# Fused block-sparse attention, top-2 expert attention and token/channel mixer on one core: the guard of the softmax sums, the first key loads, and the scaling of half the queries are rearranged

## The chip, the cores and the metric

The kernel runs on one core of one Trainium2 chip. The metric is the device time of one execution in microseconds. Before the change it is 440.44 us (median of 3 runs, 440.24 to 440.9). All data is float32, and the tolerance is tight enough that the large products are computed as three passes over a high and a low part of each operand.

## The reference

Three stages run one after the other on two batch entries (B = 2, 768 tokens, 8 heads of 64).

```python
# 1: each token attends to its neighbours and to one summary per block of 32 keys
k_sum = k.reshape(B, H, nb, block, D).max(axis=3)          # nb = 24, block = 32
v_sum = v.reshape(B, H, nb, block, D).mean(axis=3)
scores_l = scale * q @ k.T          # kept where |i - j| < 16, else -1e9
scores_s = scale * q @ k_sum.T + log(block)
a = exp(concat(scores_l, scores_s) - rowmax)
a = a / (sum(a) + 1e-9)
x = a @ concat(v, v_sum)
# 2: four experts of causal attention over x, top 2 of 4 by a gate, each projected and summed
# 3: a mixer over tokens (768 -> 256 -> 768), added, then over channels (512 -> 1536 -> 512), added
```

`scale` is 1/8, a power of two, so it is exact wherever it is applied: on the keys or on the queries.

## The kernel before

The program is written engine by engine; the order of the text is the order on each engine, and semaphores are the only coupling. There are five instruction streams: PE (matmul), DVE (vector), ACT (scalar), POOL (GpSimd) and SP, which issues nearly all DMAs.

**Attention, first stage.** For each batch entry `b` there are 12 steps `u`. Steps 0 to 5 take the six tiles of 128 queries for the first two pairs of heads (pairs 0 and 1, `q = 0`), steps 6 to 11 the same tiles for pairs 2 and 3 (`q = 1`). One step goes through:

- `a_scores` on PE: mask, then `QT` (queries, transposed) against `KW`. `KW[:, pair, window, :]` holds for every window of 64 queries its 96 neighbouring keys and the 24 block maxima, already multiplied by `scale`.
- `a_maxima` on DVE (L1464): the negated row maximum `nmaxA`.
- `a_exps` on ACT (L1192): four exponentials, each with its row sum in `sumA`.
- `a_maxima` again on DVE, one step later: `denA` = `sumA` + 1e-9 (L1469), then its reciprocal (L1475).
- `normalise` on POOL (L601): `PA` times the reciprocal, 128x480.
- `a_transpose` on PE, then `a_to_sbuf` to `PTA` (on ACT for even steps, on DVE for odd, L1482), `a_values` on PE, `a_x_hi` on ACT and `a_x_lo` on DVE (L1488) for the high and low part of the result.

The function `sequence` of each engine interleaves these with a counter `k`: at `k` PE does the scores of step `k`, the transpose of step `k - 3` and the values of step `k - 4`.

**Who builds `KW`.** In the first batch entry the windows of pairs 0 and 1 are copied and scaled on ACT (`first_windows`, L1201) and their block maxima come from DVE (`half_of_key_maxima`, L1606, on halves of the tokens); pairs 2 and 3 are scaled on POOL (`key_window`, L633), three pieces each, placed between the `normalise` calls by the table `KEY_COPIES`, and their maxima are written by DVE (`key_maxima` L1615, `fill_maxima` L1624). In the second entry pairs 0 and 1 are done on POOL during the expert stage of the first entry. `COPY_BEHIND` says after which `normalise` POOL copies block means into `VW` (L651), and `PACED` after which it splits the first weight matrix (`split_step`, L613 and L620).

**The start.** SP loads both halves of pair 0's keys, ACT's queue both halves of pair 1's; then come the first tile of queries, more queries, the keys of pair 2 and the values for the block means (`VT`), all from SP. PE warms up with 12 matmuls on `ident_b`, which POOL has built by then.

The expert stage, the token mixer and the channel mixer are not touched, except that POOL has two more instructions in the expert stage of the first entry.

Of the kernel before, what the change touches and what calls it, by code (L numbers as in the profile page):

```python
# [15 lines left out]
P = 128  # L16
# [13 lines left out]
KC = WK + NB  # L30
# [53 lines left out]
N_WARM = 12  # L84
# [9 lines left out]

MEANS_AT = 8

PACED = (5, 5, 7, 7, 8, 8)
# [38 lines left out]
def program(nc, qT_d, kT_d, vw_d, vT_d, wq_d, wk_d, wv_d, wo_d, tok1_d, tok2_d, ch1_d, ch2_d, out_d):  # L136
    with ExitStack() as ctx:
# [23 lines left out]
        sumA = sb("sumA", [P, 4, 4], F32)  # L161
# [13 lines left out]
        gate_s = sb("gate_s", [P, 2, TQ], F32)  # L175
        US1 = [None] * TQ
# [115 lines left out]
        c_mask = sem("c_mask"); c_rows = sem("c_rows")  # L292
# [17 lines left out]
        a_zero = sem("a_zero")  # L310
        a_kfirst = sem("a_kfirst"); a_kfill0 = sem("a_kfill0"); a_kfill = sem("a_kfill")
# [50 lines left out]
        def windows_by(b, q, i):  # L362

            return (2 * b + q - 1) * 6 + (4 + i if b == 0 else 2 * i + 2)

# [43 lines left out]
        def _(sp):  # L409
# [45 lines left out]
            for half in range(2):  # L455
                load_half_of_keys(sp, 0, half)
# [96 lines left out]
        def _(pool):  # L553
# [70 lines left out]
            def key_window(b, r, i):  # L624

                if i == 0:
# [6 lines left out]
                pool.tensor_scalar(KW[:, r, 4 * i:4 * i + 4, 0:WK], windows(r, 4 * i), SCALE, None,  # L633
                                   ALU.mult).then_inc(a_kwin, 1)
# [75 lines left out]
            for b in range(B):  # L710
# [25 lines left out]
                for t in range(TQ):  # L736
# [20 lines left out]
        def _(pe):  # L757
# [4 lines left out]
            pe.wait_ge(c_pool, 2)  # L762
            for _ in range(N_WARM):
                mm(bank[0], ident_b[:, :], ident_b[:, :].unsqueeze(1).broadcast_to([P, 4, P]), True, True)
# [4 lines left out]
            def a_scores(b, u):  # L769
# [10 lines left out]
                if t % 2 == 0:  # L780
# [16 lines left out]
                for j in range(2):  # L797
                    pair = 2 * q + j
                    if b + u == 0:
                        pe.wait_ge(*((a_kfirst, 1) if j == 0 else (a_kfill0, 1)))  # L800
# [323 lines left out]
            for k in range(3):  # L1124
                a_scores(0, k)
                for _ in range(WARM_BEHIND[k]):
                    mm(ps_o[:, :], ident_b[:, :], ident_b[:, :].unsqueeze(1).broadcast_to([P, 4, P]), True, True)
# [58 lines left out]
        def _(act):  # L1186
            def a_exps(b, u):
# [3 lines left out]
                for j in range(4):  # L1191
                    last = act.activation(PA[:, u % NPA, j, :], ps_s[u % 2][:, j % 2, (j // 2) * KC:(j // 2 + 1) * KC],  # L1192
                                          ACT.Exp, bias=nmaxA[:, u % 4, j:j + 1],
                                          accum_out=sumA[:, u % 4, j:j + 1])
                last.then_inc(a_exp, 1)

            def first_windows(i):
                for r in range(2):
# [207 lines left out]
            for half in range(2):  # L1406
# [463 lines left out]
```

## Time and profile before

| | |
|---|---|
| median of 3 runs | 440.44 us |
| the profiled execution's own time | 440.58 us |
| its span | 438.7 us |
| PE busy | 427.5 us, 97% |
| DVE busy | 291.0 us, 66% |
| ACT busy | 227.6 us, 52% |
| POOL busy | 144.1 us, 33% |

The shares are averages over stages with different limits. In the page's forty slices, slice 1 (the first 11 us) and the slices up to about 33 us are those where PE is least busy while DVE and ACT are at 7 to 9 tenths; after them PE is at 9 tenths almost throughout. The granted TensorE clock is at full speed in all forty slices. The profiled execution took 1.9 us more than its span; that part lies outside what the trace shows.

### The profile page before, as it was taken

Reading aid. Unit: us, or ns where it says so; the run is one execution under the profiler, and the core shown is the slowest. Engines: PE = TensorE matmul, PEld = TensorE weight load, DVE = VectorE, ACT = ScalarE, POOL = GpSimd, SP = SyncE. Lnnn points to the kernel's source line nnn. Section 1 sums busy time; section 2 is a strip of 40 time slices with the busy share of each in tenths; the row PEclk is TensorE's granted clock in tenths of the full one; section 3 lists DMA queues with packets and bytes.
Section 4 is the critical chain, followed back from the end, with each engine's and each line's share of the span. In section 5 each row is a group of like instructions: output and inputs, shape, how many; then the busy total and the mean of one; then the engine's idle time right before and its main releaser. Section 6 shows DMA issues by size and latency. Waiting matters only on the chain.

```text
span 438.7 us, 8549 instructions
## 1 busy us (share of the span) xinstructions
PE 427.5 (97%) x3327; PEld 364.5 (83%) x3327; DVE 291.0 (66%) x518; ACT 227.6 (52%) x581; POOL 144.1 (33%) x162
## 2 busy tenths in 40 slices
PE   7889999999999999999999999999999999999996
PEld 3669996887767799878877998998898999889885
DVE  4983569786478535776867875876765765575353
ACT  6895567774259736876856353434443233323120
POOL 5898927000038510001195464333122022200000
PEclk9999999999999999999999999999999999999999
DMA  8954370000870500000033013113113152301103
GB/s 282 367 203 139 108 289 0 1 2 1 291 293 13 164 6 2 0 1 1 11 105 127 1 49 96 49 48 97 48 49 96 70 184 83 97 0 49 48 0 145
DMA packets 14799, 39.66 MB, mean 90 GB/s; under 512 B 1656, under 2 KB 3368, under 8 KB 14760
## 3 DMA queue, kind: packets, MB, share of 16 engines
q1 hardware_dynamic: 14328, 38.60, 26.3%
q8 instruction: 27, 0.44, 0.4%
q10 hardware_dynamic: 432, 0.52, 0.4%
q14 instruction: 12, 0.10, 0.1%
HBM read 33.56 MB, written 4.72 MB: 87 GB/s over the span
## 4 chain that ended last, share of the span: by engine, by line
PE 87%; DVE 6%; ACT 4%; issue 2%; DMA 1%; SPq 0%; DVEq 0%
PE ps_s L759 35%; PE ps_o L759 19%; PE ps_x L759 15%; PE ps_t L759 11%; PE ps_t L941 4%; ACT PA L1192 3%; DVE nmaxA L1464 1%; DMA KP<-in_kT 1%; DVE PTA L1482 1%; DVE vsum L1630 1%; PE ps_x L958 1%; PE ps_t L835 1%; DVE denA L1469 1%; DVE XT_l L1488 0%; PE ps_s L1032 0%
## 5 line engine op out<-in xcount | busy, mean ns | idle before, releaser
L1443 ACT ACTIVATE HID_h<-HID_raw 128x384 fp32r<-128x384 f32 x48 | 25.1, 525 | 72.4 <-DVE HID_raw L1799 32.1
L704 POOL TENSOR_TENSOR W_raw<-W_raw 128x256 f32<-128x256 f32 x11 | 11.7, 1067 | 98.2 <-DMA W_raw<-in_ch 88.2
L601 POOL TENSOR_TENSOR PA<-PA,denA 128x480 f32<-128x480 f32 x24 | 23.8, 990 | 49.4 <-DVE denA L1475 49.3
L1192 ACT ACTIVATE PA<-ps_s,nmaxA 128x120 f32<-128x120 f32 x96 | 33.7, 382 | 9.9 <-DVE nmaxA L1464 9.8
L759 PE MATMUL ps_s<-C_h,HID_l 128*128 128x512 f32 x96 | 37.8, 393 | 0.0
L759 PE MATMUL ps_s<-C_l,HID_h 128*128 128x512 f32 x96 | 37.7, 393 | 0.0
L759 PE MATMUL ps_s<-C_h,HID_h 128*128 128x512 f32 x96 | 37.7, 392 | 0.0
L1558 DVE TENSOR_REDUCE nmaxM<-ps_s 128x1 f32<-128x640 f32 (+5 forms) x28 | 26.7, 955 | 12.8 <-PE ps_s L759 12.7
L1788 DVE SCALAR_TENSOR_TENSOR HID_l<-HID_raw,HID_h 128x384 fp32r<-128x384 f32 x48 | 28.0, 587 | 10.7 <-ACT HID_h L1443 8.4
L1264 ACT ACTIVATE PM<-ps_s,nmaxM 128x128 f32<-128x128 f32 (+5 forms) x48 | 30.1, 633 | 5.6 <-DVE nmaxM L1558 5.3
L759 PE MATMUL ps_o<-V_h,W_h 128*128 128x384 f32 x96 | 32.8, 342 | 0.1
L759 PE MATMUL ps_o<-V_h,W_l 128*128 128x384 f32 x96 | 32.4, 338 | 0.0
L759 PE MATMUL ps_o<-V_l,W_h 128*128 128x384 f32 x96 | 32.3, 337 | 0.0
L1664 DVE TENSOR_TENSOR W_l<-W_raw,W_h 128x1792 fp32r<-128x1792 f32 x12 | 26.1, 2179 | 5.4 <-ACT W_h L1329 5.4
L1437 ACT ACTIVATE U<-ps_o 128x384 f32<-128x384 f32 x12 | 5.9, 492 | 40.0 <-PE ps_o L759 40.0
L759 PE MATMUL ps_x<-V_h,W_h 128*128 128x384 f32 x72 | 24.3, 338 | 0.0
L759 PE MATMUL ps_x<-V_l,W_h 128*128 128x384 f32 x72 | 24.2, 336 | 0.0
L759 PE MATMUL ps_x<-V_h,W_l 128*128 128x384 f32 x72 | 24.2, 336 | 0.0
L941 PE MATMUL ps_t<-ident,PM 128*128 128x128 f32 x168 | 23.3, 275 | 0.9 <-issue 0.4
L1569 DVE COPY PTM<-ps_t 128x512 f32<-128x512 f32 x28 | 19.1, 683 | 7.0 <-PE ps_t L941 6.8
L759 PE MATMUL ps_s<-KH,QS 128*128 128x512 f32 (+3 forms) x64 | 23.6, 374 | 0.0
L1795 DVE TENSOR_TENSOR U<-ps_x,U 128x384 f32<-128x384 f32 x12 | 6.7, 556 | 24.6 <-PE ps_x L759 24.6
(257 smaller groups left out, 1266.0 us busy)
## 6 DMA issues: line engine op xcount, KB each, us to landing
VW<-in_vw SPq DMA_DIRECT2D x12, 512.0 KB, 7.7
W_raw<-in_ch SPq DMA_DIRECT2D x12, 512.0 KB, 3.5
C_raw<-in_ch SPq DMA_DIRECT2D x12, 512.0 KB, 3.9
VT<-in_vT SPq DMA_DIRECT2D x8, 384.0 KB, 7.6
out_x<-US SPq DMA_DIRECT2D x11, 256.0 KB, 2.0
QT<-in_qT SPq DMA_DIRECT2D x7, 384.0 KB, 6.8
KP<-in_kT SPq DMA_DIRECT2D x6, 384.0 KB, 7.0
raw<-in_tok SPq DMA_DIRECT2D x4, 384.0 KB, 3.1
```

The lines of the kernel that those rows point to most:

```text
L601: pool.tensor_tensor(PA[:, u % NPA, :, :], PA[:, u % NPA, :, :], denA[:, u % 2, 1, :].unsqueeze(2).broadcast_to([P, 4, KC]), ALU.mult).the ...
L704: pool.tensor_tensor(W[S3], W[A11], W[A21], ALU.subtract).then_inc(w_sum, 1)
L759: return pe.matmul(out, lhsT, rhs, start=start, stop=stop)
L941: last = pe.transpose(ps_t[:, at_ // 512, at_ % 512:at_ % 512 + P], PM[:, u % 3, at_:at_ + P], ident[:, :])
L1192: last = act.activation(PA[:, u % NPA, j, :], ps_s[u % 2][:, j % 2, (j // 2) * KC:(j // 2 + 1) * KC], ACT.Exp, bias=nmaxA[:, u % 4, j:j + ...
L1264: last = act.activation(PM[:, u % 3, part], ps_s[u % 2][:, :, :].rearrange("p a c -> p (a c)")[:, part], ACT.Exp, bias=nmaxM[:, t, e:e + 1 ...
L1443: act.activation(*own(s, n, half), ACT.Relu).then_inc(g_hi, 1)
L1558: dve.tensor_reduce(nmaxM[:, t, experts[0]:experts[0] + n], ps_s[u % 2][:, :, :].rearrange("p a c -> p (a c)")[:, 0:n * stride] .rearrange ...
L1569: dve.tensor_copy(PTM[u % 3][:, 0:width], ps_t[:, 0, 0:width]).then_inc(m_pt0, 1)
L1664: dve.tensor_tensor(W_l[i][:, :, :, :], W_raw[i][:, :, :, :], W_h[i][:, :, :, :].bitcast(F32), ALU.subtract).then_inc(w_lo, 1)
L1788: dve.scalar_tensor_tensor(HID_l[s % 2][:, n, part], quarter(s, i), 0.0, HID_h[s % 2][:, n, part].bitcast(F32), ALU.max, ALU.subtract).the ...
L1795: dve.tensor_tensor(U2[:, :], Y, U1[:, :], ALU.add).then_inc(g_u2, 1)
```

## The change

Seven edits, in the order of the program:

- **Guard.** `sumA` gets a second column that is set to 1e-9 once; `sumA + 1e-9` is now a sum over two columns (`tensor_reduce`) and no longer a `tensor_scalar`.
- **Keys of the first pairs by halves on both queues.** SP loads the first halves of pairs 0 and 1, ACT's queue the second halves. ACT scales the first window piece of pair 0, writes pair 0's block maxima, and only then scales pair 1's first piece. PE waits for each pair's piece apart.
- **Queries of pairs 2 and 3 scaled, their keys copied.** `KW` of pairs 2 and 3 is a plain copy (on POOL and, for the block maxima, on DVE). The factor goes into `QT[:, 1]`, in two halves of 128x768: on DVE in the first entry (at `k` = 5 and 8), on POOL in the second (in the expert stage of the first).
- **POOL's order.** `KEY_COPIES`, `COPY_BEHIND` and `PACED` move.
- **Warm-up.** A tile `warm`, set by DVE's first instruction, takes the place of `ident_b`, and there are 11 matmuls and no longer 12.

```diff
-KEY_COPIES = (((2, 0, -1), (2, 1, -1), (2, 2, 0), (3, 0, 2), (3, 1, 4), (3, 2, 6)),
+KEY_COPIES = (((2, 0, -1), (2, 1, -1), (2, 2, -1), (3, 0, 3), (3, 1, 4), (3, 2, 4)),
-COPY_BEHIND = (1, 3)
+COPY_BEHIND = (2, 3)
-N_WARM = 12
+N_WARM = 11
+SCALED_AT = (5, 8)
-PACED = (5, 5, 7, 7, 8, 8)
+PACED = (5, 5, 6, 7, 8, 8)
...
-        sumA = sb("sumA", [P, 4, 4], F32)
+        sumA = sb("sumA", [P, 4, 4, 2], F32)
...
-            for half in range(2):
-                load_half_of_keys(sp, 0, half)
+            for r in range(2):
+                load_half_of_keys(sp, r, 0)
...
+                if r < 2:
+                    pool.tensor_scalar(KW[:, r, 4 * i:4 * i + 4, 0:WK], windows(r, 4 * i), SCALE, None,
+                                       ALU.mult).then_inc(a_kwin, 1)
+                else:
+                    pool.tensor_copy(KW[:, r, 4 * i:4 * i + 4, 0:WK], windows(r, 4 * i)).then_inc(a_kwin, 1)
+
+            def scale_queries(b, half):
+                pool.wait_ge((ld_qf, ld_q)[half][1], b * 16 + 16)
+                part = QT[:, 1, half * GT:(half + 1) * GT, :, :].rearrange("p t j s -> p (t j s)")
+                pool.tensor_scalar(part, part, SCALE, None, ALU.mult).then_inc(a_qs, 1)
...
+                    if b < B - 1 and t in (3, 5):
+                        scale_queries(b + 1, t // 2 - 1)
...
-            pe.wait_ge(c_pool, 2)
+            pe.wait_ge(c_warm, 1)
...
                 if t == 0:
-                    pe.wait_ge(*((ld_qt, 16) if b + q == 0 else (ld_qf[q], b * 16 + 16)))
+                    pe.wait_ge(*((ld_qt, 16) if b + q == 0 else queries_by(b, q, 0)))
...
                 if t == GT:
-                    pe.wait_ge(ld_q[q], b * 16 + 16)
+                    pe.wait_ge(*queries_by(b, q, 1))
...
-            for half in range(2):
-                load_half_of_keys(act, 1, half)
+            for r in range(2):
+                load_half_of_keys(act, r, 1)
...
-            first_windows(0)
+            first_windows(0, (0,))
 
             act.wait_ge(a_ksum, 1)
             act.activation(KW[:, 0, :, WK:KC], ksum[:, 0, :].unsqueeze(1).broadcast_to([P, NW, NB]), ACT.Copy,
                            scale=SCALE).then_inc(a_kfirst, 1)
+            first_windows(0, (1,))
...
-                    dve.tensor_scalar(denA[:, before % 2, 0, :], sumA[:, before % 4, :], 1e-9, None,
-                                      ALU.add).then_inc(a_den, 1)
+                    dve.tensor_reduce(denA[:, before % 2, 0, :], sumA[:, before % 4, :, :], AX.X, ALU.add).then_inc(a_den, 1)
...
+            def scale_queries(half):
+                dve.wait_ge((ld_qf, ld_q)[half][1], 16)
+                part = QT[:, 1, half * GT:(half + 1) * GT, :, :].rearrange("p t j s -> p (t j s)")
+                dve.tensor_scalar(part, part, SCALE, None, ALU.mult).then_inc(a_qs0, 1)
...
+                    if b == 0 and k in SCALED_AT:
+                        scale_queries(SCALED_AT.index(k))
...
+            dve.memset(warm[:, :], 1.0).then_inc(c_warm, 1)
             dve.memset(denA[:, 0, 0, 0:1], 0.0)
+            dve.memset(sumA[:, :, :, 1], 1e-9)
```

`queries_by` gives the semaphore that says the queries are ready: the load's own for pairs 0 and 1, that of the scaling (`a_qs0` in the first entry, `a_qs` in the second) for pairs 2 and 3.

Two places show how the instructions move. The first is DVE in the first batch entry, from the low part of step 0's result (`XT_l`, at `k` = 5) on; `vsum` are the sums of the values of pair 2, `nmaxA` is then the maximum of step 6, the first step that reads the scaled queries. Before:

```order
L1488 TENSOR_TENSOR XT_l<-ps_o,XT_h 128x2x128
L1630 TENSOR_REDUCE vsum<-VT 128x24
L1464 TENSOR_REDUCE nmaxA<-ps_s 128x2x2
L1469 TENSOR_SCALAR denA<-sumA 128x4
L1475 RECIPROCAL denA<-denA 128x4
L1482 COPY PTA<-ps_t 120x512
```

and now:

```order
L1511 TENSOR_TENSOR XT_l<-ps_o,XT_h 128x2x128
L1656 TENSOR_SCALAR QT<-QT 128x768
L1661 TENSOR_REDUCE vsum<-VT 128x24
L1488 TENSOR_REDUCE nmaxA<-ps_s 128x2x2
L1493 TENSOR_REDUCE denA<-sumA 128x4
L1498 RECIPROCAL denA<-denA 128x4
L1505 COPY PTA<-ps_t 120x512
```

The scaling of the first half of the queries stands between the low part and the value sums, and the guard is a reduction.

The second is POOL in the first batch entry, from the first pieces of pair 2's keys on (`PA` is `normalise`, `VW` the copy of the means, `wv_h` and `wv_l` the split of the first weights). Before:

```order
L633 TENSOR_SCALAR KW<-KP 128x4x96 x2
L601 TENSOR_TENSOR PA<-PA,denA 128x480
L633 TENSOR_SCALAR KW<-KP 128x4x96
L601 TENSOR_TENSOR PA<-PA,denA 128x480
L651 COPY VW<-VS 24x512
L601 TENSOR_TENSOR PA<-PA,denA 128x480
L633 TENSOR_SCALAR KW<-KP 128x4x96
L601 TENSOR_TENSOR PA<-PA,denA 128x480
L651 COPY VW<-VS 24x512
```

and now:

```order
L649 COPY KW<-KP 128x4x96 x3
L613 TENSOR_TENSOR PA<-PA,denA 128x480 x3
L671 COPY VW<-VS 24x512
L613 TENSOR_TENSOR PA<-PA,denA 128x480
L649 COPY KW<-KP 128x4x96
L671 COPY VW<-VS 24x512
L613 TENSOR_TENSOR PA<-PA,denA 128x480
L649 COPY KW<-KP 128x4x96 x2
```

All three pieces of pair 2 stand ahead of the first `normalise`, so the first three `normalise` calls follow one another; the first piece of pair 3 stands behind the fourth, and its other two behind the fifth.

## Rows read from the trace of the kernel before

**Rows 1.** The page, the chain that ended last, by engine.

```profile
PE 87%; DVE 6%; ACT 4%; issue 2%; DMA 1%; SPq 0%; DVEq 0%
```

**Rows 2.** The chain in order of time, first 52 us: start us, us, what.

```profile
24.12 1.48 ACT PA L1192 x8
...
33.51 1.56 PE ps_s L759 x12
```

**Rows 3.** Timeline of DVE, first entry: start us, us, instruction, [idle before <-releaser].

```profile
5.43 1.47 DVE L1606 TENSOR_REDUCE ksum<-KP 128x12 f32<-128x384 f32 x3 [0.35 <-DMA KP<-in_kT]
6.93 0.31 DVE L1624 TENSOR_SCALAR KW<-ksum 128x288 f32<-128x288 f32 x1
...
9.59 0.95 DVE L1630 TENSOR_REDUCE vsum<-VT 128x24 f32<-128x768 f32 x1 [0.56 <-DMA VT<-in_vT]
...
10.87 0.66 DVE L1464 TENSOR_REDUCE nmaxA<-ps_s 128x4 f32<-128x480 f32 x1
```

**Rows 4.** The same timeline further on, to the last step.

```profile
13.22 0.95 DVE L1469 TENSOR_SCALAR denA<-sumA 128x4 f32<-128x4 f32 x1
...
15.25 0.80 DVE L1624 TENSOR_SCALAR KW<-ksum 128x288 f32<-128x288 f32 x1
...
16.54 0.15 DVE L1469 TENSOR_SCALAR denA<-sumA 128x4 f32<-128x4 f32 x1
...
18.79 0.64 DVE L1464 TENSOR_REDUCE nmaxA<-ps_s 128x4 f32<-128x480 f32 x1
...
19.54 0.18 DVE L1475 RECIPROCAL denA<-denA 128x4 f32<-128x4 f32 x1
19.63 0.40 DVE L1488 TENSOR_TENSOR XT_l<-ps_o,XT_h 128x256 fp32r<-128x256 f32 x1
...
20.80 0.65 DVE L1464 TENSOR_REDUCE nmaxA<-ps_s 128x4 f32<-128x480 f32 x1
...
26.66 0.41 DVE L1488 TENSOR_TENSOR XT_l<-ps_x,XT_h 128x256 fp32r<-128x256 f32 x1
```

**Rows 5.** Timeline of POOL, first entry.

```profile
13.15 0.99 POOL L601 TENSOR_TENSOR PA<-PA,denA 128x480 f32<-128x480 f32 x1
...
15.85 1.23 POOL L633 TENSOR_SCALAR KW<-KP 128x384 f32<-128x384 f32 x1
...
22.89 1.18 POOL L613 CAST wv_h<-raw 128x520 fp32r<-128x520 f32 x2
```

**Rows 6.** Timeline of ACT, first entry: the exponentials of steps 4 and 6.

```profile
16.65 0.36 ACT L1192 ACTIVATE PA<-ps_s,nmaxA 128x120 f32<-128x120 f32 x1 [0.56 <-DVE nmaxA L1464]
...
21.49 0.36 ACT L1192 ACTIVATE PA<-ps_s,nmaxA 128x120 f32<-128x120 f32 x1 [0.27 <-DVE nmaxA L1464]
```

**Rows 7.** Timeline of PE: the warm-up, step 9's mask, the values of step 7.

```profile
1.52 4.85 PE L759 MATMUL ps_s<-ident_b 128*128 128x512 bf16 x12 [1.52 <-POOL ident_b L563]
...
26.83 0.30 PE L759 MATMUL ps_s<-mask_m,ident_b 64*64 64x240 bf16 x4
...
32.23 0.70 PE L759 MATMUL ps_x<-PTA,VW 120*64 120x64 f32 x16 [0.17 <-DVE XT_l L1488]
```

**Rows 8.** Timeline of DVE, second entry.

```profile
133.82 0.94 DVE L1624 TENSOR_SCALAR KW<-ksum 128x288 f32<-128x288 f32 x1
```

**Rows 9.** Timeline of POOL, second entry.

```profile
132.48 1.16 POOL L633 TENSOR_SCALAR KW<-KP 128x384 f32<-128x384 f32 x1
133.61 0.98 POOL L601 TENSOR_TENSOR PA<-PA,denA 128x480 f32<-128x480 f32 x1
```

**Rows 10.** Timeline of ACT, second entry: the exponentials of step 5.

```profile
135.36 0.36 ACT L1192 ACTIVATE PA<-ps_s,nmaxA 128x120 f32<-128x120 f32 x1 [0.32 <-DVE nmaxA L1464]
```

**Rows 11.** Timeline of POOL, expert stage of the first entry.

```profile
67.47 6.85 POOL L633 TENSOR_SCALAR KW<-KP 128x384 f32<-128x384 f32 x6
```

**Rows 12.** Timeline of DVE in the same stage.

```profile
70.76 0.18 DVE L1573 TENSOR_SCALAR denM<-sumM 128x4 f32<-128x4 f32 x1
...
79.58 0.82 DVE L1558 TENSOR_REDUCE nmaxM<-ps_s 128x1 f32<-128x640 f32 x1 [1.19 <-PE ps_s L759]
```

More of the change, by code:

```diff
@@ L175, in program @@
         gate_s = sb("gate_s", [P, 2, TQ], F32)
+        warm, _ = at("warm", [P, P], BF16, place[0])
         US1 = [None] * TQ
@@ L291, in program @@
         c_pool = sem("c_pool")
-        c_mask = sem("c_mask"); c_rows = sem("c_rows")
+        c_warm = sem("c_warm"); c_mask = sem("c_mask"); c_rows = sem("c_rows")
         ld_qt = sem("ld_qt")
@@ L310, in program @@
         a_zero = sem("a_zero")
+        a_qs0 = sem("a_qs0"); a_qs = sem("a_qs")
         a_kfirst = sem("a_kfirst"); a_kfill0 = sem("a_kfill0"); a_kfill = sem("a_kfill")
@@ L364, in windows_by, with queries_by @@
             return (2 * b + q - 1) * 6 + (4 + i if b == 0 else 2 * i + 2)
+        def queries_by(b, q, half):
+            if q == 0:
+                return ((ld_qf, ld_q)[half][q], b * 16 + 16)
+            return (a_qs0 if b == 0 else a_qs, half + 1)
         def windows(r, w):
@@ L759, in mm @@
                 return pe.matmul(out, lhsT, rhs, start=start, stop=stop)
-            pe.wait_ge(c_pool, 2)
+            pe.wait_ge(c_warm, 1)
             for _ in range(N_WARM):
-                mm(bank[0], ident_b[:, :], ident_b[:, :].unsqueeze(1).broadcast_to([P, 4, P]), True, True)
+                mm(bank[0], warm[:, :], warm[:, :].unsqueeze(1).broadcast_to([P, 4, P]), True, True)
             pe.wait_ge(c_pool, N_MASK)
@@ L776, in a_scores @@
                 if t == 0:
-                    pe.wait_ge(*((ld_qt, 16) if b + q == 0 else (ld_qf[q], b * 16 + 16)))
+                    pe.wait_ge(*((ld_qt, 16) if b + q == 0 else queries_by(b, q, 0)))
                 if b + q == 0 and t == 1:
                     pe.wait_ge(ld_qf[q], 16)
-                if t % 2 == 0:
+                if t % 2 == 0 and b + u > 0:
                     pe.wait_ge(*((a_kwin0, t + 2) if b + q == 0 else (a_kwin, windows_by(b, q, t // 2))))
                 if t == GT:
-                    pe.wait_ge(ld_q[q], b * 16 + 16)
+                    pe.wait_ge(*queries_by(b, q, 1))
                 for half in range(2):
@@ L799, in a_scores @@
                     if b + u == 0:
+                        pe.wait_ge(a_kwin0, j + 1)
                         pe.wait_ge(*((a_kfirst, 1) if j == 0 else (a_kfill0, 1)))
@@ L1126, in _ @@
                 for _ in range(WARM_BEHIND[k]):
-                    mm(ps_o[:, :], ident_b[:, :], ident_b[:, :].unsqueeze(1).broadcast_to([P, 4, P]), True, True)
+                    mm(ps_o[:, :], warm[:, :], warm[:, :].unsqueeze(1).broadcast_to([P, 4, P]), True, True)
             pe.wait_ge(c_pool, N_IDENT)
@@ L1193, in a_exps, with first_windows @@
                                           ACT.Exp, bias=nmaxA[:, u % 4, j:j + 1],
-                                          accum_out=sumA[:, u % 4, j:j + 1])
+                                          accum_out=sumA[:, u % 4, j, 0:1])
                 last.then_inc(a_exp, 1)
-            def first_windows(i):
-                for r in range(2):
+            def first_windows(i, pairs=range(2)):
+                for r in pairs:
                     if i < 2:
@@ L1404, in sequence @@
                         a_first_means(b + 1)
-            for half in range(2):
-                load_half_of_keys(act, 1, half)
+            for r in range(2):
+                load_half_of_keys(act, r, 1)
             act.wait_ge(a_zero, 1)
-            act.activation(sumA[:, 3, 0:1], denA[:, 0, 0, 0:1], ACT.Exp)
+            act.activation(sumA[:, 3, 0, 0:1], denA[:, 0, 0, 0:1], ACT.Exp)
             act.wait_ge(c_pool, N_MASK)
@@ L1623, in fill_maxima @@
                         dve.wait_ge(st_u[t], b * 16)
-                dve.tensor_scalar(KW[:, r, :, WK:KC], ksum[:, r, :].unsqueeze(1).broadcast_to([P, NW, NB]),
-                                  SCALE, None, ALU.mult).then_inc(a_kfill0, 1)
+                maxima = ksum[:, r, :].unsqueeze(1).broadcast_to([P, NW, NB])
+                if r < 2:
+                    dve.tensor_scalar(KW[:, r, :, WK:KC], maxima, SCALE, None, ALU.mult).then_inc(a_kfill0, 1)
+                else:
+                    dve.tensor_copy(KW[:, r, :, WK:KC], maxima).then_inc(a_kfill0, 1)
+            def scale_queries(half):
+                dve.wait_ge((ld_qf, ld_q)[half][1], 16)
+                part = QT[:, 1, half * GT:(half + 1) * GT, :, :].rearrange("p t j s -> p (t j s)")
+                dve.tensor_scalar(part, part, SCALE, None, ALU.mult).then_inc(a_qs0, 1)
             def value_sums(b, pairs):
```

2 lines of the change are left out of this document (removed).

## Prediction

> **What bounds the kernel now.** I read the page first: PE makes up 87% of the chain that ended last [rows 1]. So a gain elsewhere is worth something only where that chain is not on PE. The chain in order of time says where: up to about 33.5 us it hops between DVE and ACT, with PE in short pieces; from the row at 33.51 on it is PE in pieces of many matmuls [rows 2]. The second batch entry repeats the attention stage from about 130 us on [rows 8 to 10]. The change touches little but these two stretches. The timelines then say who waits for whom. ACT's exponentials wait for DVE's maximum at 16.65 (0.56 us) and at 21.49 (0.27) [rows 6]; from 24.12 on the chain is on ACT for 1.48 us and more at a time [rows 2]. The reader is to see a stage that DVE bounds up to about 24 us and ACT after that, with PE close behind both.
>
> **The wait inside DVE.** The guard of the sums works on 4 numbers per partition. At 16.54 it takes 0.15 us, at 13.22 it takes 0.95 [rows 4]. Just ahead of the slow one POOL started its TENSOR_TENSOR on PA, at 13.15 for 0.99 [rows 5], and the guard ended at 14.17, as that ended. The block maxima show the same: 0.31 at 6.93 [rows 3], 0.80 at 15.25 [rows 4], 0.94 at 133.82 [rows 8] behind POOL's TENSOR_TENSOR at 133.61 [rows 9]. But at 16.54 POOL was in its TENSOR_SCALAR on KW (15.85, for 1.23) [rows 5], and DVE did not wait. So a short DVE tensor_scalar on SBUF waits for a POOL TENSOR_TENSOR to end, and hardly for a POOL TENSOR_SCALAR. The Trainium skill (SBUF — State Buffer, "Who interferes with whom") says that DVE's two-port modes, which tensor_scalar and copy enter, share a port pair with GpSimd that is held for a whole instruction, and that a tensor_reduce never contends on trn2; the slow row agrees, and no row here shows a reduction of this size against POOL.
>
> **Start: keys by halves, warm-up.** DVE waits 0.35 us for the second half of pair 0 and only then runs three reductions, to 6.91 [rows 3]. With both halves of pair 0 first on their queues the wait goes, and the first maximum of the scores comes some 0.4 us earlier. What is late next: vsum at 9.59, which waits for the transfer of VT [rows 3]. It is issued as before, so it lands as before. Behind it stand only the guard, the reciprocal and the maximum of step 2: 9.59 + 0.86 (a reduction of 0.95 lets the next start some 0.09 before its end, as 19.54 with 0.18 does for 19.63 [rows 4]) + 0.20 + 0.10 = 10.75, where it now starts at 10.87 [rows 3]. So 0.4 becomes 0.1. The warm-up starts some 0.5 us earlier and has one matmul of 4.85/12 = 0.40 us less [rows 7]; it ends about 0.9 earlier and PE waits for queries and keys instead. It costs and gives nothing; bounds are 0 and, if PE were slow afterwards, a few tenths.
>
> **First entry, relief up to step 5.** The guard at 13.22 loses 0.95 - 0.15 = 0.80. The block maxima at 15.25 lose up to 0.80 - 0.31 = 0.49; POOL will then run the three `normalise` in a row, which leaves a wait of about 0.1. So the maximum of step 4 is ready some 1.3 us earlier. ACT can use only part: its exponentials of step 3 come just 0.1 earlier, so it gains that and the 0.56 it waits at 16.65 [rows 6], and the guard of step 3 needs these exponentials. I carry forward that the maximum of step 5, now at 18.79 [rows 4], starts at 18.1, 0.7 earlier. I price the reduction as guard like the tensor_scalar, 0.16 (bounds 0.1 and 0.25, the latter as a reduction should not cost more than the 0.31 of a 288-element operation [rows 3]). POOL's plain copy of a key piece is not in the trace; its nearest row is the cast of 2 x 520 elements in 1.18, that is 0.59 each or about 0.45 for 384, against 1.16 to 1.23 now [rows 5, 9]. It frees POOL of 0.7 us for each of 12 pieces. POOL waits for reciprocals, so that only ends its work earlier.
>
> **First entry, the two scalings on DVE.** From 0.15 for 4 elements and 0.31 for 288, 768 elements take 0.15 + 764 x 0.16/284 = 0.58 us (upper bound 0.95, the 768-element reduction [rows 3]). The first stands behind XT_l of step 0, which with the 0.7 gain starts at 18.95, so it is issued at 19.26. Its reciprocal ended at 19.03, and POOL, which has less to do now, starts `normalise` at once and holds DVE's tensor_scalar as at 13.22, until about 19.9. The scaling ends at 20.5. PE's scores of step 6 wait for it (`a_qs0`) and take 0.8; behind them in PE's queue stand the transpose of step 3 and the values of step 2, whose readers have 0.5 us or more to spare. Behind the scaling on DVE stands vsum, 0.86, which covers the scores. The maximum of step 6 starts at 21.3, now 20.80 [rows 4]: the lead of 0.7 has become a lag of 0.5. ACT's wait at 21.49 of 0.27 [rows 6] was there already, so its exponentials come 0.5 later and stay 0.45 later. The second scaling stands behind XT_l of step 3, now 26.66 for 0.41 [rows 4]: issued at 26.97 + 0.3 = 27.3, held by `normalise` of step 7 to about 27.4, ended at 28.0. PE's scores of step 9, now 26.83 [rows 7], wait for it: 1.2 later. PE runs without a gap from 26.83 to the values of step 7 but for 0.17 [rows 7], so 1.0 us of lag arrives at 33.51. If neither scaling were held, the same walk gives 20.62 for step 6's maximum and 27.25 for step 9's scores: +0.42 - 0.17 = +0.25. If both are held for the full 0.99 it is about +1.5. I take +1.0.
>
> **Second entry.** The scaling is on POOL, in the expert stage. What remains is relief: the block maxima at 133.82 wait 0.94 - 0.31 = 0.63 for a `normalise` that began at 133.61 because a key piece of 1.16 from 132.48 stood before it [rows 8, 9]. With the piece at 0.45, `normalise` starts at 133.36, 0.25 earlier, and DVE is free 0.25 earlier. ACT waits 0.32 there [rows 10], so 0.25 fits. I take -0.25; bounds 0 and -0.63.
>
> **Expert stage.** POOL's two scalings cost up to 2.3 us each, twice a key piece (768 elements against 384; six pieces take 6.85, 1.14 each [rows 9, 11]). Nobody on POOL is queued behind them until the second entry's first `normalise`. While POOL was in six such TENSOR_SCALARs from 67.47 for 6.85 us [rows 11], a DVE guard at 70.76 took 0.18 [rows 12]. So 0.
>
> **Sum.** +1.0 (first entry, start included) - 0.25 (second) + 0 = +0.75. On the profiled execution, 440.58, that is 441.3; it stood 0.14 above the median, so 441.2 against 440.44.
>
> **Rivals.**
> - *The relief outweighs* (faster). The scalings find the port free, since `normalise` waits longer than I think, and PE makes up the 0.42 at step 9 in slack, as its chain there is really ACT's: then the 0.18 lead of step 6 holds, 0.2 more comes from the lost wait of guards later on, and the second entry gives up to 0.6. Against it: the stall at 13.22 and at 133.82 has just this order of instructions. It decides where the maximum of step 6 starts before 20.80. Time about 439.6, up to 440.1.
> - *POOL's scalings block DVE in the expert stage* (slower still). Worked out: one of 2.3 us some 1 us behind the six pieces, from about 75.2, would hold the next two-input or two-port DVE instruction to 77.5; DVE has 1.19 us of idle ahead of 79.58 [rows 12], so PE loses 0.5 to 1, and the second one a few tenths: +0.7, that is 441.9. Against it stands the 0.18 at 70.76 [rows 12]. The skill's section cited above says that any GpSimd instruction holds the pair for its whole length; by that rule this rival would be the forecast, and the row at 70.76 disagrees.
> - *Nothing reaches the chain* (no change). ACT and PE bound the stage so tightly that relief and cost both end in waits; ACT has only 0.1 to 0.6 of idle per step. 440.4.
> - A smaller one, within the first: the halves on two queues land no earlier than before, which takes 0.1.
>
> **How the numbers follow.** Forecast 441.2 with 0.48, its own range 440.7 to 441.9; relief outweighs 0.28; POOL blocks 0.12; nothing 0.12. A measurement of this kernel tells about 0.2%, 0.9 us, from no change: the bounds are 439.6 and 441.3. The forecast gives 0.21 slower, 0.26 within and 0.01 faster; the first rival 0.15 faster and 0.13 within; the second 0.12 slower; the third 0.12 within. Together faster 0.16, within 0.51, slower 0.33. The range reaches from the lower end of the first rival, 439.4, to just above the second, 442.0.
>
> **What would show it.** On DVE's timeline: no guard above 0.25 us; the scalings at 0.58 alone and at 1.0 or more where `normalise` runs; vsum still at 9.59 behind DMA. The maximum of step 6 at 21.3 and PE's scores of step 9 at 28.0 would show the cost, and the first long PE piece at about 34.5 instead of 33.51. If that piece comes before 33.5, the cost of the scalings is what I have wrong; if DVE shows long rows near 75 to 77 and 87 to 89 us, the second rival holds.

## The result, and the profile after

The changed kernel takes 444.01 us (median of 4 runs, 443.49 to 444.09), the kernel before 440.67 us beside it (4 runs, 440.24 to 441.09). The ratio is 1.0073, 95% interval 1.0056 to 1.0091: slower by 3.3 us, outside the range of 439.4 to 442.0. The profiled execution took 444.08 us, its span is 442.3 us against 438.7.

Three rows of PE cut the span into stages: the first product with `wv` of the first entry (it ends that entry's attention), the first scores of the second entry, and the first `wv` of the second entry. All times here and in the table of experiments are starts in us.

| | first wv | second entry's first scores | second entry's wv | span |
|---|---|---|---|---|
| before | 33.39 | 120.53 | 149.11 | 438.7 |
| after | 37.40 | 124.58 | 152.93 | 442.3 |
| difference | +4.01 | +4.05 | +3.82 | +3.6 |

So the whole loss is in the first 37 us, the expert stage (87.14 before, 87.18 after) is unchanged, and the second entry is 0.23 us shorter (28.58 to 28.35).

The chain that ended last, by engine, then its longest piece in the first entry (start us, us, what):

```profile
PE 89%; DVE 4%; ACT 3%; DMA 2%; issue 1%; SPq 1%; DVEq 0%
```
```profile
4.00 7.67 DMA QT<-in_qT
```

PE has 2% more of it than in [rows 1], and a load of queries that lands at 11.67 is on it, which wasn't among the long pieces before. The scores of step 3, which wait for it, begin at 11.80, where they began at 11.55.

PE of the changed kernel, from the values of step 1 to the last scores ahead of full speed, then step 9 and the first `wv` (start us, us, instruction, [idle before <-releaser]):

```profile
17.68 0.73 PE L781 MATMUL ps_x<-PTA,VW 120*64 120x64 f32 x16
21.19 0.41 PE L781 MATMUL ps_s<-mask_m,ident_b 64*64 64x240 bf16 x4 [2.77 <-DVE QT L1656]
...
21.43 1.08 PE L781 MATMUL ps_s<-KW,QT 64*64 64x120 f32 x16
22.44 1.11 PE L858 MATMUL ps_t<-ident,PA 128*120 128x128 f32 x4
23.48 1.18 PE L781 MATMUL ps_o<-PTA,VW 120*64 120x64 f32 x16
...
27.75 0.30 PE L781 MATMUL ps_s<-mask_m,ident_b 64*64 64x240 bf16 x4
...
31.16 0.30 PE L781 MATMUL ps_s<-mask_m,ident_b 64*64 64x240 bf16 x4 [0.85 <-DVE QT L1656]
...
37.40 0.37 PE L781 MATMUL ps_s<-wv_h,XT_h 128*128 128x260 f32 x1
```

The scores of step 6 begin at 21.19, behind 2.77 us in which PE had nothing to do, and wait for `QT` from DVE's scaling. Then the same work takes longer: the transpose 1.11 us and the values 1.18, where ahead of the wait the values took 0.73. The windows of the same stretch say why (stretch, its length, busy us of PE, PEld, DVE, ACT and POOL with counts, granted TensorE clock, DMA share, GB/s):

```profile
20.00:21.00 1.00, 0.00 (x0) 0.00 (x0) 1.00 (x2) 0.90 (x5) 1.00 (x2) 0.80 1.00 223
21.00:27.00 6.00, 5.81 (x74) 4.42 (x76) 4.55 (x11) 1.83 (x10) 2.85 (x5) 0.50 0.84 310
27.00:28.00 1.00, 1.00 (x28) 0.93 (x32) 0.24 (x1) 1.00 (x4) 0.99 (x2) 0.79 0.00 0
```

The granted clock fell to 0.50, the 1.2 GHz level, late in the wait and stayed there from 21 to 27 us of steady work. From 21.19 to 27.75 PE did six units (scores, transpose and values of one step, and the same of the next) in 6.56 us. Against the kernel before, the scores of step 6 are 2.2 us late at 21.19, and those of step 8 are 4.3 us late at 27.75 (23.44 before): about half of the lag arises in this slow stretch, and no more is added behind it. The other three executions of the changed kernel aren't traced, but all four have a mean clock below full speed, 0.992 twice and 0.996 twice. On the page the row of the granted clock shows it as one 7 in the third of forty slices:

```profile
PEclk9979999999999999999999999999999999999999
```

DVE of the changed kernel: value sums, guard, block maxima, maximum of step 5, the first scaling, maximum of step 6, the second scaling.

```profile
9.75 0.95 DVE L1661 TENSOR_REDUCE vsum<-VT 128x24 f32<-128x768 f32 x1 [1.25 <-DMA VT<-in_vT]
...
13.20 0.15 DVE L1493 TENSOR_REDUCE denA<-sumA 128x4 f32<-128x8 f32 x1
...
14.44 0.40 DVE L1651 COPY KW<-ksum 128x288 f32<-128x288 f32 x1
...
18.45 0.65 DVE L1488 TENSOR_REDUCE nmaxA<-ps_s 128x4 f32<-128x480 f32 x1
...
19.61 1.32 DVE L1656 TENSOR_SCALAR QT<-QT 128x768 f32<-128x768 f32 x1
...
22.57 0.66 DVE L1488 TENSOR_REDUCE nmaxA<-ps_s 128x4 f32<-128x480 f32 x1 [0.78 <-PE ps_s L781]
...
30.37 0.64 DVE L1656 TENSOR_SCALAR QT<-QT 128x768 f32<-128x768 f32 x1
```

and POOL beside them: the three plain key pieces, and the `normalise` of step 4.

```profile
8.84 1.40 POOL L649 COPY KW<-KP 128x384 f32<-128x384 f32 x3 [3.07 <-issue]
...
19.53 0.98 POOL L613 TENSOR_TENSOR PA<-PA,denA 128x480 f32<-128x480 f32 x1 [0.46 <-DVE denA L1498]
```

Against [rows 4], the guard is no longer held (0.15 where it took 0.95), and the block maxima take 0.40 and not 0.80. The first scaling is issued 0.08 us behind POOL's `normalise` and ends at 20.93, 0.4 behind its end at 20.51. The second, issued at 30.37, meets only the last 0.23 us of a `normalise` (29.61 for 0.99), again ends 0.4 behind that one's end, and takes 0.64. POOL's next instruction, a split that took 0.73 at 27.95, then takes 1.05 at 30.56: now POOL is held by DVE. The maximum of step 6 waits for PE's late and slow scores and comes at 22.57, where it came at 20.80.

In the second entry the block maxima take 0.74 us, where they took 0.94 [rows 8], as `normalise` starts earlier ahead of them (DVE, then POOL, of the changed kernel):

```profile
137.87 0.74 DVE L1651 COPY KW<-ksum 128x288 f32<-128x288 f32 x1
```
```profile
137.46 0.99 POOL L613 TENSOR_TENSOR PA<-PA,denA 128x480 f32<-128x480 f32 x1 [0.46 <-DVE denA L1498]
```

### The profile page after: what moved, and what is told of

Its sections match the earlier page's. It is cut to its first block, busy times and chain, and to the rows that moved or that the text cites. A ratio compares the mean times of both kernels' runs of the same rounds, so it can differ in the third digit from the quotient of the medians.

```text
span 442.3 us, 8555 instructions
## 1 busy us (share of the span) xinstructions
PE 430.0 (97%) x3326; PEld 366.6 (83%) x3326; DVE 290.9 (66%) x522; ACT 228.1 (52%) x581; POOL 140.9 (32%) x164
## 3 DMA queue, kind: packets, MB, share of 16 engines
HBM read 33.56 MB, written 4.72 MB: 87 GB/s over the span
## 4 chain that ended last, share of the span: by engine, by line
PE 89%; DVE 4%; ACT 3%; DMA 2%; issue 1%; SPq 1%; DVEq 0%
PE ps_s L781 36%; PE ps_o L781 19%; PE ps_x L781 15%; PE ps_t L781 11%; PE ps_t L964 4%; ACT PA L1215 2%; DMA QT<-in_qT 2%; PE ps_t L858 2%; PE ps_x L981 1%; DVE PTA L1505 1%; DVE nmaxA L1488 1%; ACT PTA L1249 0%; DVE QT L1656 0%; PE ps_s L1055 0%; DVE XT_l L1511 0%
```

## Experiments

**Theory A:** the cost is PE's wait for the scaling that POOL holds, and the fall of the clock behind that wait. **Theory B:** the wait alone, the clock being a side effect. **Theory D:** DVE's time, 1.3 us and 0.6 us more in a stage that DVE bounds. Each kernel was compared with the kernel before in the same session (medians there 440.62, 440.66 and 440.72 us).

| kernel | us | ratio to before, 95% interval | first wv |
|---|---|---|---|
| changed, PE kept busy in the wait | 442.10 | 1.0021 (1.0004 to 1.0038) | 35.56 |
| changed, no factor on queries | 440.91 | 1.0002 (0.9987 to 1.0016) | 34.11 |
| changed, scaling ahead of the reciprocal | 440.08 | 0.9987 (0.9963 to 1.0010) | 35.23 |
| the same again | 441.38 | 1.0010 (0.9991 to 1.0030) | 33.56 |
| no factor, scalings into an unread tile | 441.17 | 1.0008 (0.9995 to 1.0022) | 33.77 |
| changed, scores of step 6 last | 442.69 | 1.0043 (1.0031 to 1.0055) | 36.13 |
| before, guard alone | 440.36 | 0.9992 (0.9984 to 1.0001) | 33.07 |
| no factor, POOL's old order | 440.54 | 0.9996 (0.9983 to 1.0010) | 32.40 |
| that, with the factor in the second entry | 440.03 | 0.9985 (0.9976 to 0.9994) | 33.63 |
| changed, tiles scaled on POOL | 447.61 | 1.0155 (1.0125 to 1.0184) | 38.64 |
| before, guard and factor in the second entry | 439.69 | 0.9972 (0.9959 to 0.9986) | 32.63 |

The landmark is of one execution. The first value sums, which wait for the landing of `VT`, began between 9.08 and 9.94 us in these traces, and two kernels with the same first entry (no factor with POOL's old order, and that with the factor in the second entry) have landmarks 1.2 us apart. So the medians decide, and the landmark only explains. The kernel before is not free of falls of the clock either: beside these kernels it ran 83 times, and the five executions with a mean clock of 0.995 or 0.996 took 442.85 to 443.28 us, 2.2 to 2.7 above the medians.

**PE kept busy.** Twelve matmuls on the constant tile `warm` ahead of the scores of step 6 and three ahead of those of step 9.

```diff
+FILL = {6: 12, 9: 3}
...
+                if b == 0 and u in FILL:
+                    for _ in range(FILL[u]):
+                        mm(ps_s[u % 2][:, 0, :], warm[:, :], warm[:, :].unsqueeze(1).broadcast_to([P, 4, P]), True, True)
```

> The changed kernel with idle-time matmuls: ahead of the scores of step 6 PE does 12 warm-up matmuls, ahead of those of step 9 it does 3, before it waits for the scaled queries. Nothing else moves. Theory A (the clock): PE's wait of 2.77 us for the first scaling lets its granted clock fall to half from about 20 to 27 us, and that costs some 2.7 of the 4.1 us that the first entry lost. Then the granted clock stays at 1.00, scores 6 still start near 21.1, and the time is 441.3 (440.9 to 441.9). Theory B (the wait alone; the slow stretch lies beside DVE and ACT work): the clock stays up too, but the time stays at 443.5 to 444.2.

Of this kernel, PE's fillers, and the window from 22 us on:

```profile
18.40 2.76 PE L782 MATMUL ps_s<-warm 128*128 128x512 bf16 x12
```
```profile
22.00:28.00 6.00, 5.07 (x98) 3.63 (x98) 5.60 (x16) 4.10 (x19) 4.53 (x6) 1.00 0.84 319
```

The scaling is still held (19.67 for 1.32) and the scores of step 6 begin at 21.09, as late as ever. Only the clock is different: 1.00. The six units that took 6.56 us take 3.89 (21.09 to 24.98). By the medians that is worth 444.01 - 442.10 = 1.9 us. The result lies between the two expectations, 0.2 above the upper end of A's and 1.4 below B's, so B alone falls; some 1.5 us over the kernel before remain. Part of that is the price of the fillers themselves. The three ahead of step 9 came too late to fill a wait:

```profile
27.98 0.64 DVE L1660 TENSOR_SCALAR QT<-QT 128x768 f32<-128x768 f32 x1
```
```profile
28.57 0.82 PE L782 MATMUL ps_s<-warm 128*128 128x512 bf16 x3
29.33 0.30 PE L782 MATMUL ps_s<-mask_m,ident_b 64*64 64x240 bf16 x4
```

The scaling ended at 28.62, and the scores began at 29.33. By these rows the fillers cost about 0.6 us (an estimate), so that the clock is worth rather more than 1.9 and the wait itself rather less than 1.5.

**No factor on the queries.** The factor is back on all keys; guard, start, and POOL's new order stay.

```diff
-                    pool.tensor_copy(KW[:, r, 4 * i:4 * i + 4, 0:WK], windows(r, 4 * i)).then_inc(a_kwin, 1)
+                pool.tensor_scalar(KW[:, r, 4 * i:4 * i + 4, 0:WK], windows(r, 4 * i), SCALE, None,
+                                   ALU.mult).then_inc(a_kwin, 1)
...
-            return (a_qs0 if b == 0 else a_qs, half + 1)
+            return ((ld_qf, ld_q)[half][q], b * 16 + 16)
```

> The changed kernel without its query part: the keys of pairs 2 and 3 are scaled again as before, no scaling of the queries. Guard, start, warm-up and POOL's new order stay. Theories A and B both put the whole loss on the scaling of the queries: 439.4 to 440.4, 440.0 my value (a little under the kernel before, whose guard waits are gone), clock at 1.00. Theory C (another part costs as well: POOL's new order, or the later first waits of PE on the new start): over 441.

440.91 us: without the scaled queries the loss is gone. But it is 0.5 above the range that I expected, and the relief brought nothing either. On PE and POOL of this kernel one reads why:

```profile
13.36 0.65 PE L851 MATMUL ps_t<-ident,PA 128*120 128x128 f32 x4 [0.75 <-POOL PA L611]
```
```profile
8.91 3.44 POOL L643 TENSOR_SCALAR KW<-KP 128x384 f32<-128x384 f32 x3 [3.14 <-issue]
12.32 2.87 POOL L611 TENSOR_TENSOR PA<-PA,denA 128x480 f32<-128x480 f32 x3
```

With pieces of 1.15 us, three of them ahead of the first `normalise` start it at 12.32, and PE's first transpose waits. POOL's new order suits only the plain copies.

**Scaling ahead of the reciprocal.** In the first entry each scaling stands behind the guard and ahead of the reciprocal that releases POOL's next `normalise`; `then` is `scale_queries` at `k` = 5 and 8.

```diff
                     dve.tensor_reduce(denA[:, before % 2, 0, :], sumA[:, before % 4, :, :], AX.X, ALU.add).then_inc(a_den, 1)
+                if then is not None:
+                    then()
```

> The changed kernel with each of the two DVE scalings moved two instructions up, ahead of the reciprocal that lets POOL start normalise. If POOL's TENSOR_TENSOR is what held the first scaling, it now takes 0.64 and not 1.32 us and ends near 19.9 instead of 20.9; scores 6 start 1.0 earlier. By theory A the clock may then still fall, but less: 442.0 (441.0 to 443.0). By theory B 443.0, exactly the 1.0 less. If it is not POOL that held it, it still takes 1.3 us, ends near 20.6 and the time stays above 443.5.

> The changed kernel with each of the first entry's scalings ahead of the reciprocal and not behind it, again, since its 10 runs lay between 439.7 and 443.4 and its profiled run at 441.8, near the upper end. If the place of the scaling decides: median 439.8 to 440.5, first scaling 0.55 to 0.65 us, and the first piece of wv about 33.5 in a profiled run near the median (35.23 in the one at 441.8). If the first result was a lucky draw: 441 or more.

DVE, then PE, of the first of the two, whose profiled execution took 441.77 us:

```profile
19.06 0.55 DVE L1658 TENSOR_SCALAR QT<-QT 128x768 f32<-128x768 f32 x1
```
```profile
19.87 0.30 PE L781 MATMUL ps_s<-mask_m,ident_b 64*64 64x240 bf16 x4 [1.48 <-DVE QT L1658]
```

The same instruction takes 0.55 us where it took 1.32: POOL's `normalise` starts at 19.85, behind it. It also starts 0.55 earlier, as it stands ahead of two more instructions; of the 1.32 us by which it ends sooner, 0.77 is the hold and the rest its place. The second scaling was still held: it took 0.84 in both profiled executions, here at 25.68 behind a split on POOL that ran from 25.37 for 0.74. PE's wait ahead of step 6 falls to 1.48 us and in both profiled executions the clock stayed at full speed. The two medians, 440.08 and 441.38, differ by more than I expected. Both lie below the 442.0 that I had first expected, and 440.08 below its range (441.0 to 443.0) as well; but it was partly a lucky draw: of the 12 executions of the repeat, the four with a mean granted clock of 0.995 or 0.996 took 442.48 to 443.46 us, the eight at 0.999 or 1.0 took 439.90 to 441.80. With the one of 0.996 in the first ten, that is 5 of 22 executions, against 5 of 83 of the kernel before: a wait of 1.5 us there leaves the clock at risk, though no trace shows one of these five. Nor does the clock explain all of the spread: the profiled execution at 441.77 ran at full clock and has waits of 1.33 and 1.09 us on PE (at 27.45 and 34.16) which the one at 440.22 doesn't have, and the profile names nothing that PE waited for there. The earlier place, hold and position together, is worth 2.6 to 3.9 us, most of the loss.

**Scalings nobody waits for.** As the kernel without the factor, and DVE does both scalings all the same, into a tile that is not read.

```diff
-                dve.tensor_scalar(part, part, SCALE, None, ALU.mult).then_inc(a_qs0, 1)
+                dve.tensor_scalar(aside[:, :], part, SCALE, None, ALU.mult).then_inc(a_qs0, 1)
```

> The kernel of e2 with the two DVE scalings added again at their places, but written to a tile that nobody reads, so that PE does not wait for them (its output is the reference's). DVE's work is that of the changed kernel, PE's wait is gone. Theory A: what costs is PE's wait and the clock behind it: DVE's 1.3 and 0.6 us alone cost 0.2 to 0.9 over e2, 440.5. Theory D (DVE's queue is the bound and its longer work is what costs): 2 us or more over e2.

Its two scalings on DVE, one of them held:

```profile
19.90 0.56 DVE L1648 TENSOR_SCALAR aside<-QT 128x768 f32<-128x768 f32 x1
...
27.27 1.40 DVE L1648 TENSOR_SCALAR aside<-QT 128x768 f32<-128x768 f32 x1
```

The first took 0.56, as it came ahead of POOL's `normalise` of 20.13, which then took 1.17 and not 0.99. 1.96 us of DVE's time cost 441.17 - 440.91 = 0.3 us, within the noise of both. Theory D falls: what costs is who waits for the scaling.

**Scores of step 6 last.** PE does the transpose of step 3 and the values of step 2 ahead of them.

```diff
+                    late = b == 0 and k == 6
-                    if k < NU:
+                    if k < NU and not late:
                         a_scores(b, k)
...
                         a_values(b, k - 4)
+                    if late:
+                        a_scores(b, k)
```

> The changed kernel, with one difference in PE's queue: in the first entry at k = 6 the transpose of step 3 and the values of step 2 stand ahead of the scores of step 6, so PE has 1.2 us of work while DVE's scaling is held. Theory A (PE's wait of 2.77 us for the held scaling, and the halved clock behind it, are what the change costs): PE's idle time ahead of the scores of step 6 falls to 1.5 us or less, the granted clock stays at 1.00 from 20 to 30 us as it did behind the 1.48 us of wait when the scaling stood ahead of the reciprocal, the first piece of wv comes at 35.3 to 35.7 instead of 37.40, and the time is 441.5 to 442.1. If the wait of the scores decides and not what PE does in it: clock at 0.50 again, 37 or more, 443.5 or more.

PE of this kernel:

```profile
19.61 0.85 PE L781 MATMUL ps_o<-PTA,VW 120*64 120x64 f32 x16 [0.84 <-DVE XT_l L1514]
20.96 0.30 PE L781 MATMUL ps_s<-mask_m,ident_b 64*64 64x240 bf16 x4 [0.50 <-DVE QT L1659]
...
28.63 0.30 PE L781 MATMUL ps_s<-mask_m,ident_b 64*64 64x240 bf16 x4 [1.50 <-DVE QT L1659]
```

PE's 2.77 us are cut into 0.84 and 0.50, the clock stays at 1.00, and 1.3 us come back. But the start of step 6 (20.96 against 21.19) is as late as the scaling, and the second scaling is now waited for 1.50 us. The landmark, 36.13, and 442.69 us lie above what I expected (35.3 to 35.7, 441.5 to 442.1).

**Guard alone, on the kernel before.** Its edit, beside the second column of `sumA`:

```diff
-                    dve.tensor_scalar(denA[:, before % 2, 0, :], sumA[:, before % 4, :], 1e-9, None,
-                                      ALU.add).then_inc(a_den, 1)
+                    dve.tensor_reduce(denA[:, before % 2, 0, :], sumA[:, before % 4, :, :], AX.X, ALU.add).then_inc(a_den, 1)
```

> The kernel before with the guard alone: 1e-9 in a column beside the sums, a reduction over two columns. If the relief is real for the chain: no guard above 0.25 us (before 0.95 at 13.22, 0.31 to 0.48 from 25 to 31 us), the first piece of wv 0.2 to 0.6 ahead of 33.39, ratio 0.998 to 0.9995. If the relief ends in ACT's and PE's other waits, or the block maxima are held in the guard's place: within 0.1 of 33.39, ratio 1.0000.

440.36 us, ratio 0.9992: about 0.3 us, at the edge of what can be told. A guard in the middle of POOL's TENSOR_TENSORs takes 0.16 us (28.34, while POOL is in two of them from 27.36 for 1.43), where before it took 0.48 at 28.46. But the first block maxima took the guard's place in the hold, on DVE of this kernel:

```profile
14.65 0.75 DVE L1623 TENSOR_SCALAR KW<-ksum 128x288 f32<-128x288 f32 x1
```

**POOL's old order, without the factor, and with it in the second entry alone.** The first takes the three tables from the kernel before:

```diff
-KEY_COPIES = (((2, 0, -1), (2, 1, -1), (2, 2, -1), (3, 0, 3), (3, 1, 4), (3, 2, 4)),
-COPY_BEHIND = (2, 3)
-PACED = (5, 5, 6, 7, 8, 8)
+KEY_COPIES = (((2, 0, -1), (2, 1, -1), (2, 2, 0), (3, 0, 2), (3, 1, 4), (3, 2, 6)),
+COPY_BEHIND = (1, 3)
+PACED = (5, 5, 7, 7, 8, 8)
```

and the second is the changed kernel with these tables, without DVE's scalings, and with

```diff
-                if r < 2:
+                if r < 2 or b == 0:
...
-            if q == 0:
+            if q == 0 or b == 0:
```

> The changed kernel without the scaled queries (factor on all keys, as before) and with POOL's order of before, so that guard, keys by halves and warm-up are left. Without the scaled queries but with POOL's new order the ratio was 1.0002, and there three key pieces of 1.15 us each stood ahead of the first normalise, which began at 12.32 instead of 11.07. If that order took the relief away: first transpose back from 13.36 to about 12.5, first piece of wv at 33.2 or less, ratio 0.998 to 0.9993. If the start by halves itself costs (PE waits 0.65 to 0.78 for QT's load ahead of the scores of step 2): 33.6 or more, ratio 1.0003 or more.

> As the one without scaled queries and with POOL's old order, but in the second entry alone the factor is on the queries (POOL scales them in the expert stage) and the keys of pairs 2 and 3 are copied. Theory A (only the scalings that PE waits for in the first entry cost, POOL's in the expert stage cost nothing): between the two landmarks of the first entry's wv and the second entry's first scores nothing changes, and the second entry is 0.2 us shorter by the relief, 0.2 less than the kernel without it. If POOL's scalings of 2.14 us cost in the expert stage: 0.3 or more above it.

440.54 and 440.03 us. With the old order the first transpose is at 11.88, where it was at 13.36, and the landmark at 32.40, both as expected, but in an execution of 439.70 us, near the fastest of its twelve; the median, 0.9996, lies above the range that I gave (0.998 to 0.9993), and it is unclear against 440.91 with the new order. PE's wait of 0.65 to 0.78 for queries, which I put to the new start, is 0.47 here and 0.61 with the guard alone and the old start, so it goes with the landing and isn't shown to come from the start. The keys by halves bring nothing that can be told beside the guard alone (440.36). From the second entry's first scores to its first `wv` the first takes 28.55 us and the second 28.34: the 0.2 of the prediction. The stretch ahead of it, with the expert stage, takes 87.29 and 87.30 us, so POOL's two scalings in the expert stage cost nothing.

**Tiles scaled on POOL.** Six pieces of 128x256, behind the `normalise` of steps 2, 3, 4, 7, 8 and 9.

```diff
+TILES_BEHIND = (2, 3, 4, 7, 8, 9)
...
+                    if b == 0 and u in TILES_BEHIND:
+                        scale_tile(TILES_BEHIND.index(u))
```

> The changed kernel, with the factor on the first entry's queries put on by POOL, tile by tile (128x256, six of them, 0.7 us each by a third of the 2.14 us that POOL takes for 768 elements), behind the normalise of steps 2, 3, 4, 7, 8 and 9, and not by DVE. If the place on DVE (behind the reciprocal, so behind POOL's next normalise) is what costs and the moved factor itself is harmless: no wait for QT above 0.5 us ahead of the scores of step 6, clock at 1.00 from 20 to 30 us, first piece of wv at 33.5 to 34.5, time 439.9 to 440.7. If POOL is short of time in the steps from 6 on (14.0 us of work there before, now about 15.5 in 13.5 us): PE waits for POOL's PA or QT, 34.5 to 36, time 441 to 442.

The worst of all, 447.61 us, beyond both expectations. The first three pieces did what they were meant to, with no wait for them ahead of step 6 and a clock of 1.00 to 28 us. But I had placed the second half too late: PE's step 9 waits for a piece that stands behind the `normalise` of step 7 and the split of a weight. Its PE row and windows (the profiled execution took 445.25 us, the fastest of six, with a mean clock of 0.996; the other five, with 0.985 to 0.989, aren't traced):

```profile
28.32 0.30 PE L789 MATMUL ps_s<-mask_m,ident_b 64*64 64x240 bf16 x4 [2.70 <-POOL QT L660]
```
```profile
26.00:28.00 2.00, 0.00 (x0) 0.00 (x0) 0.55 (x2) 1.98 (x10) 2.00 (x3) 1.00 0.15 41
28.00:30.00 2.00, 1.68 (x27) 1.40 (x28) 0.42 (x1) 0.34 (x2) 0.88 (x2) 0.63 0.75 209
30.00:32.00 2.00, 1.66 (x19) 1.13 (x17) 0.79 (x4) 1.41 (x6) 1.41 (x2) 0.52 0.37 111
```

It is a second case of a fall behind a wait, this time for another engine: 2.70 us without work, and then a clock of 0.63 and 0.52.

**Guard and second entry, on the kernel before.** The guard's edit above and, with `scale_queries` on POOL in the expert stage as in the change,

```diff
-                pool.tensor_scalar(KW[:, r, 4 * i:4 * i + 4, 0:WK], windows(r, 4 * i), SCALE, None,
-                                   ALU.mult).then_inc(a_kwin, 1)
+                if r < 2 or b == 0:
+                    pool.tensor_scalar(KW[:, r, 4 * i:4 * i + 4, 0:WK], windows(r, 4 * i), SCALE, None,
+                                       ALU.mult).then_inc(a_kwin, 1)
+                else:
+                    pool.tensor_copy(KW[:, r, 4 * i:4 * i + 4, 0:WK], windows(r, 4 * i)).then_inc(a_kwin, 1)
```

> The kernel before with two parts of the change alone: the guard as a reduction, and the factor on the queries of pairs 2 and 3 in the second entry alone (POOL scales them in the expert stage). The keys by halves and the new warm-up are left out. Guard alone gave 0.9992, the factor in the second entry about 0.2 us more in the traces. If the two add and the start by halves brings nothing: ratio 0.9980 to 0.9990, 440.1 us, 28.3 us between the second entry's first scores and its first wv (before 28.58). If the start was worth something: 440.3 or more.

439.69 us, ratio 0.9972 (0.9959 to 0.9986), a little better than the 0.9980 to 0.9990 that I expected; the second entry's stretch is 28.36 us, as expected. It is the fastest, 1.0 us below the kernel before and 4.3 below the changed one. It leaves out the keys by halves, the new warm-up, POOL's new order and all scaling of queries that PE has to wait for.

## Why the prediction was wrong

**The step that failed** is the first scaling's: "The scaling ends at 20.5. PE's scores of step 6 wait for it (`a_qs0`) and take 0.8", with "I take +1.0" for the entry. The mechanism, DVE's scaling held by `normalise` and PE waiting, was right, and the end of the scaling was off by only 0.4 (20.93). But I carried the delay only as lateness, and put the price of PE's standing still at nothing without a reason. On PE of the kernel before:

```profile
17.54 0.73 PE L759 MATMUL ps_x<-PTA,VW 120*64 120x64 f32 x16
18.97 0.30 PE L759 MATMUL ps_s<-mask_m,ident_b 64*64 64x240 bf16 x4 [0.70 <-issue]
```

With step 6 moved from 18.97 to 20.5, its wait of 0.70 us becomes some 2.2, in a kernel whose profiled execution has none above 0.72 between 9 and 33 us and a clock at full speed. The rows show what followed: a wait of 2.77, granted clock 0.50 from 21 to 27 us, the scores that had to take 0.8 took 1.3, and six units took 6.56 us and not 3.89. The prediction named the clock only at the warm-up ("if PE were slow afterwards, a few tenths"), not at the longest wait that the change makes. Keeping the clock returned 1.9 us, out of a loss of 3.3 and a miss of 2.8 against the forecast of 441.2. What stays open is how the price goes with the length of a fall: the two executions of the changed kernel with a mean clock of 0.996 took as long (443.95 and 444.09) as the two with 0.992.

The rest, step by step:

- *Sum.* Forecast +1.0 for the first entry, measured +4.0 at the first `wv`. With the clock kept it is 442.10 - 440.62 = 1.5 us of time for the whole kernel, the late fillers included, twice the forecast of 0.75: so the clock is most of the miss and not all. The lag of PE's scores of step 6 was 2.2 and not 1.5, and it was not made up on the way: with the clock kept the first `wv` is still 2.2 late, 0.6 of it from the fillers.
- *The scaling alone.* Forecast 0.58, measured 0.55 and 0.56 where it is not held: right. The hold was to last until 19.9; but `normalise` began only at 19.53 and lasted to 20.51.
- *Relief up to step 5.* Forecast 0.7 ahead, measured 18.79 to 18.45, 0.34. The guard and the block maxima gave what I said, but DVE then waits 0.97 us for ACT's exponentials ahead of the guard at 16.38. ACT was no earlier (its exponentials of step 3 begin at 14.87, before at 14.62), as the scores of step 3 waited 0.78 for queries at 11.80, a landing that I hadn't looked at. The relief had the sign of the forecast and half its size.
- *Step 9.* Forecast 28.0, measured 31.16. The second scaling was hardly held, as forecast (0.64), but came with the lag, which was 4.3 us at step 8 already.
- *Start.* Forecast 0.1. The first maximum came 0.53 earlier (7.27 against 7.80 [rows 3]) and `vsum` waited 1.25 for `VT`, so that the maximum of step 2 came at 10.90 where it came at 10.87: swallowed whole, where I had left 0.1.
- *Guard.* Forecast 0.16, measured 0.15. *Plain key piece.* Forecast about 0.45, measured 1.40/3 to 0.50. *Second entry.* Forecast -0.25, measured -0.23.
- *Expert stage.* Forecast 0, measured +0.04 in 87 us. POOL's scalings took 2.14 us. One DVE instruction beside them, the low part `OT_l` at 79.47, took 0.85 where it takes 0.41 or 0.42 elsewhere; PE didn't notice. The rival that gave this 0.7 us falls.
- *Relief outweighs*, the rival with 0.28, fell on its condition: the first scaling found the port held. A gain is what happens once the first entry's scalings are gone: 440.03 and 439.69. *Nothing reaches the chain* fell with the 3.3 us.

## What to carry to other kernels

When a change makes PE wait, write down how long it then has no work at all, not only by how much its result is late, and add the price of the work behind it at the 1.2 GHz level: here 1.9 us or somewhat more for a wait of 2.8. An instruction that an engine waits for must not stand behind the one that starts its competitor for a port; ahead of the reciprocal the same scaling took 0.55 and not 1.32 us. And a relief is worth what the next two landings and engines leave of it; test the parts apart, since here two of them made the best kernel.

## What the runs showed of the hardware

- The granted clock fell behind 2.77 us (the changed kernel) and 2.70 us (tiles on POOL) without PE work, in the profiled executions; behind 1.48, 1.50 and 1.78 us it stayed at 1.00 in them, though the repeat of the early scaling had four executions of twelve with a lower mean clock. In the first of them the six microseconds from 21 to 27, with PE busy for 5.81, passed at 0.50 ahead of the return to 1.00. In executions without a trace a mean clock of 0.995 or 0.996 went with some 2 to 3.5 us more, in the kernel before too (5 of 83).
- A plain copy on DVE is held by POOL's TENSOR_TENSOR like a tensor_scalar (0.74 us for the 0.31 of the block maxima), and a small reduction isn't (0.15 to 0.16). DVE holds POOL the same way where it comes first: the split 1.05 us for 0.73, and `normalise` 1.17 for 0.99. The Trainium skill (SBUF — State Buffer, "Who interferes with whom") says both, that copies and tensor_scalars can enter the two-port modes and a tensor_reduce on trn2 never contends; the rows now agree on the reduction too.
- POOL copies 384 elements per partition in 0.50 us and multiplies them in 1.17: the factor costs more than the copy.
